# Attention and mixture of experts on one core: the first loads in another order and on another queue

## The reference, cut to what matters

```python
psi_rel = np.log1p(np.abs(rel))                    # rel[i, j] = i - j
psi_i = np.log1p(np.maximum(pos[:, None], 1.0))
x = (psi_rel / psi_i)[..., None]
h = np.maximum(x @ w1 + b1, 0.0)                   # hidden size 32
bias = h @ w2                                      # one value per head
scores = scale * q @ k.T + bias.transpose(2, 0, 1)[None]
attn = softmax(scores); out = attn @ v
# then: noisy gate, top 2 of 8, relu(x @ w1[e]) @ w2[e], weighted sum
```

## Time and profile before

| | us |
|---|---|
| median of three runs | 801.66 |
| the profiled execution, its own time | 800.91 |
| its span on the core | 798.7 |
| TensorE busy | 760.0 |
| VectorE (DVE) busy | 494.4 |
| ScalarE (ACT) busy | 390.6 |
| GpSimd (POOL) busy | 383.2 |

### The profile page before, as it was taken

One profiled execution on the slowest core, in us unless ns is written; L12 is line 12 of the kernel. 1 busy time (PEld: TensorE's weight loads), 2 busy tenths in 40 slices (PEclk: granted clock), 3 DMA queues, 4 the chain that ended last, 5 costly groups with the idle time before them and its releaser, 6 DMA issues.

```text
span 798.7 us, 18524 instructions
## 1 busy us (share of the span) xinstructions
PE 760.0 (95%) x6658; PEld 615.4 (77%) x6658; DVE 494.4 (62%) x1235; ACT 390.6 (49%) x836; POOL 383.2 (48%) x440
## 2 busy tenths in 40 slices
PE   4887999999999998998999999999999999999995
PEld 2335767776776665978898998998998988988984
DVE  6898999998999897875536335335344344354311
ACT  5996887888888776505334133233232232241200
POOL 0008999899899784035333324224414413423312
PEclk9998999999999999999999999999999999999998
DMA  7786443353353363219633723714804804713213
GB/s 164 218 232 145 118 127 105 108 157 107 105 158 103 88 218 134 76 30 303 192 126 58 199 88 72 223 49 79 263 4 77 262 13 83 247 26 66 41 21 45
DMA packets 51719, 98.49 MB, mean 123 GB/s; under 512 B 12736, under 2 KB 21696, under 8 KB 51648
## 3 DMA queue, kind: packets, MB, share of 16 engines
q1 hardware_dynamic: 40352, 74.55, 30.2%
q0 software_dynamic: 10720, 22.72, 14.4%
q10 hardware_dynamic: 576, 0.29, 0.2%
HBM read 66.38 MB, written 20.53 MB: 109 GB/s over the span
## 4 chain that ended last, share of the span: by engine, by line
PE 82%; DMA 6%; ACT 4%; issue 3%; DVE 3%; POOL 1%; POOLq 0%; SPq 0%; ACTq 0%; DVEq 0%
PE ps L779 27%; PE po L794 24%; PE po L691 11%; PE ps L609 8%; PE pt L636 7%; DMA out_rows<-ys,iscat 2%; DMA slab<-work 2%; PE pt L615 2%; ACT work L1338 2%; ACT work L1319 2%; PE pt L650 1%; PE pt L623 1%; DMA b1col<-in_b1c 1%; DVE ns L948 0%; POOL xg L1607 0%
## 5 line engine op out<-in xcount | busy, mean ns | idle before, releaser
L779 PE MATMUL ps<-xT,whi 128*128 128x310 f32 (+1 forms) x960 | 161.1, 306 | 3.3 <-ACT xT L1489 3.3
L794 PE MATMUL po<-whi,hT 128*128 128x512 f32 (+1 forms) x640 | 161.0, 396 | 0.1
L779 PEld LDWEIGHTS ps<-xT,whi 128*128 128x128 f32 x960 | 143.3, 190 | 4.1 <-ACT xT L1489 2.5
L1501 ACT ACTIVATE hT<-ps 128x310 fp32r<-128x310 f32 x112 | 48.2, 430 | 196.8 <-PE ps L779 180.6
L794 PEld LDWEIGHTS po<-whi,hT 128*128 128x128 f32 (+1 forms) x640 | 118.1, 188 | 25.8 <-DVE hT L1103 0.5
L1262 DVE SCALAR_TENSOR_TENSOR hT<-ps,hT 128x310 fp32r<-128x310 f32 x112 | 53.8, 481 | 133.6 <-ACT hT L1501 114.8
L1565 POOL TENSOR_SCALAR work<-work,rcp 128x576 f32<-128x576 f32 (+1 forms) x160 | 117.6, 745 | 26.5 <-DVE rcp L961 26.1
L1354 ACT ACTIVATE work<-ns,nmax 128x576 f32<-128x576 f32 (+1 forms) x160 | 123.0, 769 | 3.6 <-DVE nmax L948 3.5
L948 DVE CUSTOM_DVE_ANT_0 ns<-ps,slab 128x576 f32<-128x576 f32 (+1 forms) x160 | 119.8, 750 | 7.8 <-PE ps L609 6.4
L1607 POOL DMA_INDIRECT xg<-x_rows,igath x38 | 42.3, 1113 | 164.6 <-DVE ys L1277 73.9
L1620 POOL DMA_INDIRECT out_rows<-ys,iscat x35 | 60.4, 1727 | 95.7 <-DMA out_rows<-ys,iscat 66.0
(11 more groups left out here) (181 smaller groups left out, 1105.2 us busy)
## 6 DMA issues: line engine op xcount, KB each, us to landing
wraw<-in_mw SPq DMA_DIRECT2D x64, 512.0 KB, 6.3
slab<-work SPq DMA_DIRECT2D x36, 288.0 KB, 3.8
qraw<-in_qT SPq DMA_DIRECT2D x64, 144.0 KB, 2.8
vs<-in_v SPq DMA_DIRECT2D x32, 160.0 KB, 2.6
out_rows<-zeros SPq DMA_DIRECT2D x32, 152.0 KB
kraw<-in_kT SPq DMA_DIRECT2D x64, 72.0 KB, 2.3
x_rows<-xnat SPq DMA_DIRECT2D x8, 576.0 KB, 4.5
xg<-x_rows,igath POOLq DMA_INDIRECT x38, 7.0
```

Of the source, the lines that this page charges most:

```text
L779: mm = nc.tensor.matmul(ps[n % 4 // 2][:, n % 2, 0:w], w1s[i][pw][:, c, f * P:(f + 1) * P], x[px][:, c, :], start=j == 0 and c == 0, stop= ...
L794: mm = nc.tensor.matmul(po[0:m, (i + t) % 2, :], hT[px][:, at:at + m], w2s[i][pw][:, c, :], start=j == 0 and c == 0, stop=j == 2 and c == ...
```

## The change

The two columns are requested by GpSimd, ahead of its memsets, on a semaphore of their own, `col_loaded`, for which DVE and ACT now wait beside `c_loaded`. `c_loaded` counts the eight table pieces only. SP no longer waits for `c_loaded`. Of the requests between the tables and the copies three stay (identity, `r8raw`, `w2blk`); the twelve from L461 to L479 are issued one at a time, each behind the copy of a group: queries and keys of head 0 behind groups 4, 6, 8, 10, of head 1 behind 12, 14, 16, 18, the gates behind 20 and 22, the noise behind 24, the constants behind 26. `load_qk` for later heads does what it did.

```diff
-        CONSTS = 16 * (2 * GQ + 2)
+        CONSTS = 16 * 2 * GQ
@@ sync
-            sp.dma_start(w1col[:, :], w1c).then_inc(c_loaded, 16)
-            sp.dma_start(b1col[:, :], b1c).then_inc(c_loaded, 16)
             sp.dma_start(cst[:, 0:P], consts[:, 0:P]).then_inc(p_loaded, 16)
             sp.dma_start(r8raw[:, :], rcp8).then_inc(p_loaded, 16)
             sp.dma_start(w2blk[:, :], w2b).then_inc(w2_loaded, 16)
-            sp.wait_ge(c_loaded, CONSTS)
-            sp.dma_start(cst[:, P:C_END], consts[:, P:C_END]).then_inc(tri_loaded, 16)
...
-            load_qk(0)
-            load_qk(1)
-            for half in range(2):
+            def load_gates(half):
                 sp.dma_start(wgs[:, :, half * 16:(half + 1) * 16],
                              wg.rearrange("p (c e) -> p c e", c=H)[:, :, half * D:half * D + 16]).then_inc(c2_loaded, 16)
-            sp.dma_start(wnoise[:, :, :], noise.rearrange("p (t e) -> p t e", t=NT)).then_inc(c2_loaded, 16)
+            def load_noise():
+                sp.dma_start(wnoise[:, :, :], noise.rearrange("p (t e) -> p t e", t=NT)).then_inc(c2_loaded, 16)
             for g in range(GROUPS):
                 u, base = GROUP[g]
                 sp.wait_ge(bev_done, g + 1)
                 sp.dma_start(bias[base:base + SPREAD * (QG - 1) + 1:SPREAD, u, :, :], bst[g % NB])\
                     .then_inc(bst_moved[g % NB], 16)
+                n, part = divmod(g - 4, 8)
+                if 0 <= n < 2 and part % 2 == 0:
+                    load_q(n, part // 2) if part < 4 else load_k(n, part // 2 - 2)
+                elif n == 2 and part in (0, 2):
+                    load_gates(part // 2)
+                elif n == 2 and part == 4:
+                    load_noise()
+                elif n == 2 and part == 6:
+                    sp.dma_start(cst[:, P:C_END], consts[:, P:C_END]).then_inc(tri_loaded, 16)
@@ vector
             dve.wait_ge(c_loaded, CONSTS)
+            dve.wait_ge(col_loaded, 32)
             nc.vector.tensor_scalar(rw, rw, w1col[:, 0:1], None, ALU.mult).then_inc(rw_done, 1)
@@ scalar
             act.wait_ge(c_loaded, CONSTS)
+            act.wait_ge(col_loaded, 32)
             nc.scalar.activation(bp, bp, ACT.Copy, scale=b1col[:, 0:1]).then_inc(rw_done, 1)
@@ gpsimd
+            pool.dma_start(w1col[:, :], w1c).then_inc(col_loaded, 16)
+            pool.dma_start(b1col[:, :], b1c).then_inc(col_loaded, 16)
             nc.gpsimd.memset(zeros[:, :], 0.0).then_inc(zero_done, 1)
```

More of the change, by code:

```diff
@@ L342, in build @@
         c_loaded = sem("c_loaded")
+        col_loaded = sem("col_loaded")
         p_loaded = sem("p_loaded")
@@ L459, in _, with load_q, load_k @@
             sp.dma_start(w2blk[:, :], w2b).then_inc(w2_loaded, 16)
-            sp.wait_ge(c_loaded, CONSTS)
-            sp.dma_start(cst[:, P:C_END], consts[:, P:C_END]).then_inc(tri_loaded, 16)
+            def load_q(n, half):
+                sp.dma_start(qraw[n % 2][half * D:(half + 1) * D, :], qT[n, :, :]).then_inc(q_loaded[n % 2], 16)
+            def load_k(n, half):
+                sp.dma_start(kraw[n % 2][half * D:(half + 1) * D, :], kT[n, :, half * HALF:(half + 1) * HALF])\
+                    .then_inc(k_loaded[n % 2], 16)
             def load_qk(n):
-                if n >= 2:
-                    sp.wait_ge(q_split, n - 1)
+                sp.wait_ge(q_split, n - 1)
                 for half in range(2):
-                    sp.dma_start(qraw[n % 2][half * D:(half + 1) * D, :], qT[n, :, :]).then_inc(q_loaded[n % 2], 16)
-                if n >= 2:
-                    sp.wait_ge(k_split, n - 1)
+                    load_q(n, half)
+                sp.wait_ge(k_split, n - 1)
                 for half in range(2):
-                    sp.dma_start(kraw[n % 2][half * D:(half + 1) * D, :], kT[n, :, half * HALF:(half + 1) * HALF])\
-                        .then_inc(k_loaded[n % 2], 16)
-            load_qk(0)
-            load_qk(1)
-            for half in range(2):
+                    load_k(n, half)
+            def load_gates(half):
                 sp.dma_start(wgs[:, :, half * 16:(half + 1) * 16],
                              wg.rearrange("p (c e) -> p c e", c=H)[:, :, half * D:half * D + 16]).then_inc(c2_loaded, 16)
-            sp.dma_start(wnoise[:, :, :], noise.rearrange("p (t e) -> p t e", t=NT)).then_inc(c2_loaded, 16)
+            def load_noise():
+                sp.dma_start(wnoise[:, :, :], noise.rearrange("p (t e) -> p t e", t=NT)).then_inc(c2_loaded, 16)
             for g in range(GROUPS):
```

## The result

The changed kernel takes 806.46 us (median of 7 runs, 801.85 to 810.15) against 801.66 (7 runs): ratio 1.006, 95% interval 1.0035 to 1.0084. It is slower by more than the 0.5% that I had given 0.03, and outside my range of 796.0 to 801.4. Its profiled execution took 806.46 us with a span of 804.6.

What follows compares the result with a forecast made beforehand. The prediction took the start of attention to be set by how soon 36 groups of bias rows are through, then TensorE work. Gains 0.6 + 2.15 + 0 + 0.4 = 3.15, rounded to 3.2: 801.66 to 798.5 us, range 796.0 to 801.4.

Steps and rivals of the forecast that it cites:

- slower by more than the 0.5%: Whole kernel: a loss above 0.5%, here 4.0 us, needing the third rival beyond its own price; chance 0.03.
- The columns: Start of the bias stage: columns on GpSimd's queue, wait ends with pcol at 6.8 instead of 7.4, gain 0.6 us.
- SP out of the way: Early bias stage: ACT's 2.52 us wait at group 4 and both DVE stalls go, gain 2.15 us.
- The interleaved loads: Bias stage, groups 4 to 26: twelve loads between copies, priced at 0, covered by landing slack and a 1.1 us reserve.
- third rival: Bias stage: interleaved loads become the bound, six rounds 1.0 us longer, less 1.1 reserve, against 2.75 won; 803.8, chance 0.07.
- The tail: End of the bias stage: last copies spread out, part of DVE's 0.99 us wait at tile 4 goes, gain 0.4 us.
- my sum without the columns: Bias stage: the gains of 2.15 us (SP out of the way) and 0.4 us (the tail), loads at 0.
- Attention and experts: Behind the bias stage: attention and the expert stage should be as long as before.

Runs made afterwards that it cites:

- e1: The kernel before with only the two columns moved to GpSimd's queue: 802.92 us, ratio 1.0009.
- e2: The changed kernel with the columns back on SP's queue, so the interleaving alone: 805.96 us, ratio 1.0057.
- e4: e2 without loads between copies: queries and keys requested by SP ahead of them, gates, noise and constants by GpSimd: 801.22 us, ratio 0.9989.
- e9: The same kernel as e4, run once more: 801.73 us, ratio 0.9993.
- e3: The changed kernel with 7 staging buffers instead of 4, nothing else: 805.86 us, ratio 1.0036.
- e5: e4 plus twelve additional loads of 64 bytes per partition behind groups 4, 6, ... 26: 800.61 us, ratio 0.9996.
- e6: e4 plus twelve additional loads with the changed kernel's sizes and sources (1.38 MB), behind groups 4, 6, ... 26: 808.21 us, ratio 1.0094.
- e7: e4 with the four groups of the last row block spread over the order instead of together at the end: 801.09 us, ratio 0.9997.

## Why the prediction was wrong, by its own steps

**The columns: wrong in sign, small.** The step was that `pcol` at 6.8 would end the wait. `pcol` did end it, but at 7.67, and in e1 at 7.93. I had taken the landings of the tables as given. With the columns on SP (before, e2, e4 to e9) DVE started between 7.36 and 7.53; with them on GpSimd's queue (the changed kernel, e3, e1) at 7.70, 7.71 and 7.96. So the move costs 0.3 to 0.5 us where I had booked 0.6 of gain, and these values lie between the ends that I had set. Whether it is the column packets beside `pcol` or SP's next tables 0.94 earlier was not tried. The Trainium skill, page "DMA: Bandwidth & Descriptors", section "Issuing engines are not separate DMA queues", says that requests share the 16 DMA engines whichever engine issues them, and that issuing from several saves only the sequencer's time. The trace agrees: with the columns on a third queue the last piece of `pcol` landed at 7.67 and 7.93 instead of 6.8, and the time saved on SP gained nothing.

**SP out of the way: right, 2.15 us.** In the changed kernel the pause at group 4, the clock of 0.50 and both DVE stalls of the earlier trace rows are gone, though a new one of 0.36 us stands at 14.16, in the slow start of TensorE. The first copy went out at 13.01 and not at 12.1, because DVE started at 7.70 and not at 6.8. e4 shows the step by itself, with no DVE stall at all. Its split is 1.7 us earlier and not 2.15, above all because of the 0.7 us that DVE lost beside GpSimd's requests.

**The interleaved loads: priced at 0, measured at 7.6 us. This is the step that failed.** It said: "A group occupies the DMA engines for 0.80 x 1.30 = 1.04 us, a query load by its bytes for 0.52". The full queue of e3 has 1.20 for the copy and 0.9 to 1.3, on average 1.1, for the query load. Busy share times period is not the spacing at which copies can follow one another. So the spare time was 0.09 us per group, 2.2 over 24 groups, not 0.26 and 6.2, and the loads wanted 9.6 instead of 6.0; about half of the error is the copy and half the loads. What does not fit, 7.4 us, must go somewhere. In the changed kernel the requests of copies 4 and 28 are 37.4 us apart, before 31.3, so 6.0 more; and copy 28 landed 5.8 instead of 4.1 us after its request. e5 and e6 show the price by itself, 7.6 us between twelve short and twelve full loads. In the changed kernel it is about 7.8 by difference: 5.9 us of loss in the span, plus the 2.15 won, less the 0.3 of the start. A check could have been had from the trace of before: beside the 231 GB/s of the mid-stage stands the crowded stretch at the first copies, with 251 (windows, columns as in the earlier trace rows).

```profile
16.00:20.50 4.50, 2.40 (x36) 0.83 (x32) 4.50 (x12) 1.98 (x4) 0.00 (x0) 1.00 0.98 251
```

That leaves 9%, not 25%.

The mechanism was on my list as the third rival, with six rounds of buffers and a price of 1.0 us each; I gave it 0.07. By its own formula, with the median of 5.2 to 5.4 that came, it would have given 803.2 to 804.4 (6 x 0.9 or 1.1, less 1.1 and 2.75, on 801.66) against 806.46. It was 2 to 3 us short because it kept my 0.6 of gain at the start, which came as 0.3 of loss, and had no term for a longer tail, which took 2.4 more. My ground against it, that only four slots hold a query load, counted slots instead of adding the queue's time.

The Trainium skill, page "DMA: Bandwidth & Descriptors", section "Anatomy of one DMA — SWDGE (gpsimd) path", fits a DMA that GpSimd issues by 2.0 us plus its bytes over 436 GB/s. For 288 KB that would be 2.7 us, an estimate that does not carry over to these copies, which SP issues: no run shows one landed before 3.1 us, and in the full queue of e3 they follow one another at 246 GB/s.

**The tail: wrong in sign.** I expected a gain of 0.4, as ACT would no longer be late. ACT was late again, and the wait at tile 4 rose from 0.99 to 2.65 us; from split to tile 4 it took 10.5 us instead of 8.2. Even without interleaving the wait rose, to 1.67 in e4 and 1.21 in e9: the last copies are bound by their own service, so a bias stage that is computed earlier gives part of the gain back right there. Of the 2.6 us of my sum without the columns, 1.0 arrives at tile 4 in e4 and 0.7 in e9, so the forecast would have been too low even with the loads out of the way.

**Attention and experts** only followed, as forecast.

Open are why DVE is slower while GpSimd issues requests, what sets the moment at which TensorE's pace doubles, why the loads cost more than their bytes, and what share of the tail comes from the instruction fetches.

## What to carry to other kernels

To see whether a transfer stream has room, take the spacing at which transfers follow one another out of a full queue (a stretch behind a stall, or a run with more buffers), not busy share times period: here 1.20 us against 1.04, which turned 20% of room into 7%. In this kernel the loads that nobody needed yet were cheapest ahead of the stream (before, e4, e9), even though before they held up its first copy by 2.2 us. Between the copies they cost their queue time beyond the little that was spare, and the one large load near the end seems to have cost more than that. And a stage that ends with a stream of copies gives back part of what its compute gains until the copies gain too.

## What the runs showed of the hardware beyond expectation

- A load of 144 KB from HBM into 64 partitions cost 0.9 to 1.3 us of a full queue beside these SBUF copies, as much as some 220 to 310 KB of copy would (an estimate from e3's spacings).
- DMA share 1.07 went with 224 GB/s (changed kernel, 38 to 42 us) and 0.80 with 231 (before): with a full queue the share rose and the bytes did not.
- A landing is set by the last of 16 parts. Around a 16 KB instruction fetch (0.9 to 1.3 us on one DMA engine) that part lay up to 1.7 us behind the other 15; without loads it was back after three or four copies (before, groups 10 to 13), in the changed kernel it was still 1.1 to 1.7 behind in groups 3 to 6, until others were as late. That the fetch is the cause is inferred from the coincidence in time.
- Twelve requests of 64 bytes per partition between the copies moved the median landing by 0.2 us (3.8 in e4, 4.0 in e5) and the time not measurably.
- While GpSimd issued four DMAs (7.8 to 11.5 us in e4), three of DVE's hidden tiles took 0.84, 0.82 and 0.58 us instead of 0.52; the same in e5, e6, e7 and e9.
- TensorE's pace in its first matmuls of the bias stage doubled at 11.9 us before, 13.2 in e4 and 15.9 in e9, where the trace's first record of the granted clock (1.00) stands. e4 and e9 are one kernel.
